# An attention and two MLP stages on one core: the odd heads' state product gets a bank of its own, the first unit full triangles, the range check two slots

## The reference, cut to what matters

```python
    for t in range(S):
        state = alpha[:, :, t, :, None] * state + np.einsum('bhd,bhe->bhde', k[:, :, t], v[:, :, t])
        y[:, :, t] = np.einsum('bhd,bhde->bhe', q[:, :, t], state)
...
    x = np.ascontiguousarray(attn_out.transpose(0, 2, 1, 3)).reshape(B, S, H * D)
...
    xn = (x - mu) / np.sqrt(var + 1e-06) * g_ln
    ch = np.maximum(xn @ w_ch1, 0.0) @ w_ch2
    return (x + ch).astype(np.float32)
...
    X = np.fft.fft(x, axis=1)
    X = np.fft.fft(X, axis=2)
    mixed = np.real(X).astype(np.float32)
    u = x + mixed
```

## Time and profile before

| what | value |
|---|---|
| median of 3 runs | 779.54 us (778.01 to 780.23) |
| profiled execution, its time | 780.88 us |
| its span in the trace | 779.4 us |
| PE busy | 765.5 us, 98% |
| DVE, ACT, POOL busy | 450.4, 218.6, 54.8 us |
| stage one (attention and first MLP) | up to about 440 us |

### The profile page before, as it was taken

One profiled execution on the slowest core, in us unless ns is written; L12 is line 12 of the kernel. 1 busy time (PEld: TensorE's weight loads), 2 busy tenths in 40 slices (PEclk: granted clock), 3 DMA queues, 4 the chain that ended last, 5 costly groups with the idle time before them and its releaser, 6 DMA issues.

```text
span 779.4 us, 17212 instructions
## 1 busy us (share of the span) xinstructions
PE 765.5 (98%) x7148; PEld 740.3 (95%) x7148; DVE 450.4 (58%) x1035; ACT 218.6 (28%) x453; POOL 54.8 (7%) x110
## 2 busy tenths in 40 slices
PE   7999999999999999999999999999999999999998
PEld 7889899999999999999999999999999999999998
DVE  6787777766666665675586865347434564342422
ACT  3453242232312323124243332212221223111221
POOL 1000000000000000000003100300012000300000
PEclk9899999999999999999999999999999999999999
DMA  9352304041130410443023511030003000000000
GB/s 248 99 151 66 97 33 139 32 108 61 52 88 32 119 62 32 138 144 113 21 92 102 193 51 55 27 102 31 1 32 102 30 0 30 0 0 31 1 31 30
DMA packets 29827, 54.10 MB, mean 69 GB/s; under 512 B 1916, under 2 KB 24700, under 8 KB 29756
## 3 DMA queue, kind: packets, MB, share of 16 engines
q1 hardware_dynamic: 29756, 53.10, 22.1%
HBM read 43.65 MB, written 13.37 MB: 73 GB/s over the span
## 4 chain that ended last, share of the span: by engine, by line
PE 89%; DVE 4%; issue 4%; ACT 1%; DMA 1%; POOL 0%; SPq 0%; POOLq 0%; DVEq 0%; ACTq 0%
PE h L97 13%; PE h L99 12%; PE acc L99 12%; PE h L98 12%; PE acc L97 12%; PE acc L98 12%; PE side_bank L1452 3%; PE side_bank L1463 2%; PE side_bank L1472 2%; PE side_bank L1402 2%; PE side_bank L98 2%; PE side_bank L99 2%; PE side_bank L97 1%; PE side_bank L1414 1%; PE side_bank L1385 1%
## 5 line engine op out<-in xcount | busy, mean ns | idle before, releaser
L171 DVE SCALAR_TENSOR_TENSOR hT_low<-h,hT_high 128x384 fp32r<-128x384 f32 (+1 forms) x204 | 108.5, 532 | 187.5 <-ACT hT_high L166 187.3
L97 PE MATMUL h<-xnT_high,w_high 128*128 128x384 f32 (+1 forms) x612 | 208.5, 341 | 1.2 <-DVE hT_low L171 0.9
L99 PE MATMUL h<-xnT_high,w_low 128*128 128x384 f32 (+1 forms) x612 | 199.9, 327 | 0.0
L98 PE MATMUL h<-xnT_low,w_high 128*128 128x384 f32 (+1 forms) x612 | 199.6, 326 | 0.0
L166 ACT ACTIVATE hT_high<-h 128x384 fp32r<-128x384 f32 (+1 forms) x204 | 96.4, 472 | 354.6 <-PE h L99 354.0
L97 PE MATMUL acc<-w_high,hT_high 128*128 128x384 f32 x576 | 194.3, 337 | 0.0
L99 PE MATMUL acc<-w_high,hT_low 128*128 128x384 f32 x576 | 193.3, 336 | 0.0
L98 PE MATMUL acc<-w_low,hT_high 128*128 128x384 f32 x576 | 192.8, 335 | 0.0
L97 PEld LDWEIGHTS h<-xnT_high,w_high 128*128 128x128 f32 x612 | 115.2, 188 | 5.7 <-issue 0.9
L98 PEld LDWEIGHTS h<-xnT_low,w_high 128*128 128x128 f32 x612 | 115.5, 189 | 0.0
L99 PEld LDWEIGHTS h<-xnT_high,w_low 128*128 128x128 f32 x612 | 115.2, 188 | 0.0
(11 more groups left out here) (135 smaller groups left out, 764.6 us busy)
## 6 DMA issues: line engine op xcount, KB each, us to landing
stage<-w_dram SPq DMA_DIRECT2D x24, 384.0 KB, 3.6
x_scratch<-x_unit SPq DMA_DIRECT2D x8, 576.0 KB, 3.0
a_in<-alpha_dram SPq DMA_DIRECT2D x6, 672.0 KB, 5.1
q_in<-q_dram SPq DMA_DIRECT2D x6, 672.0 KB, 7.4
k_in<-k_dram SPq DMA_DIRECT2D x6, 672.0 KB, 6.8
v_in<-v_dram SPq DMA_DIRECT2D x6, 576.0 KB, 3.8
xb<-x_scratch SPq DMA_DIRECT2D x4, 576.0 KB, 4.2
xb<-x_turned SPq DMA_DIRECT2D x4, 576.0 KB, 6.9
```

The source lines that it names most:

```text
L97: pe.matmul(out, wh, xh, start=start, stop=False)
L98: pe.matmul(out, wh, xl, start=False, stop=False)
L99: return pe.matmul(out, wl, xh, start=False, stop=stop)
L171: dve.scalar_tensor_tensor(out=self.hT[1][:, j % H_SLOTS, 0:u.cols], in0=self.hps[j % H_BANKS][:, 0:u.cols], scalar=0.0, in1=self.hT[0][:, ...
```

## The change

1. **Chunks of all units but the first.** The masked scores by v (now `outputs_within`) all go to bank BSC, and stand behind the increments, one slot earlier. The products of state and q (now `outputs_carried`) stay in the output slot, alone: even heads add to BSC, odd heads start in BY. ACT copies BSC in one instruction, and DVE adds BY to the odd heads (`add_odd`), which raises `x_odd`. Scores of the next chunk wait for it too. The first chunk of a sequence multiplies with the zero state, where it left that product out.
2. **First unit.** The chunk isn't halved: scores are 128 by 128 with a full triangle (`causal`), increments go to one bank, chunk 0 has no state product, and chunk 1 does its scores ahead of its transposes. `first_half_state` is gone.
3. **Range check** in two slots: `check_above` in `range_slot`, `check_below` in the slot after it, behind that slot's `copy_y`. The slot of ONE[1] becomes 5.
4. **DVE order.** For ONE[2] `mask` and `next_state` come ahead of `prepare`. In the last unit of stage one, `dve_low` of slot 0 comes ahead of the residual of the unit before.

```diff
-ONE[1].scores, ONE[1].increments, ONE[1].outputs, ONE[1].range_slot = (4, 7), (5, 8), (6, 9), 7
+ONE[1].scores, ONE[1].increments, ONE[1].outputs, ONE[1].range_slot = (4, 7), (5, 8), (6, 9), 5
...
-            probs = [sb1(f"probs{i}", [P, PAIRS, SUB]) for i in range(2)]
+            probs = [sb1(f"probs{i}", [P, PAIRS, P]) for i in range(2)]
...
+                if u.first():
+                    for two in range(2):
+                        op = act.activation(odd_even(to)[:, two, :, :], of_pairs(first_y_bank(two)[:, 0:PAIRS * D]),
+                                            ACT.Copy)
+                else:
+                    op = act.activation(to, bank[BSC][:, 0:DM], ACT.Copy)
...
                 if slot == u.range_slot:
-                    check_range(u)
+                    check_above(u)
+                if slot == u.range_slot + 1:
+                    check_below(u)
...
+            def add_odd(u, c):
+
+                dve.wait_ge(x_ready, u.base + c + 1)
+                odd = odd_even(x_rows(u)(c))[:, 1, :, :]
+                dve.tensor_tensor(odd, of_pairs(bank[BY][:, 0:PAIRS * D]), odd, ALU.add).then_inc(x_odd, 1)
...
-                if slot > 1:
+                if slot > 1 and u.n != 2:
                     prepare()
                 if slot in u.scores:
                     mask(u, u.scores.index(slot))
                 if slot in u.increments:
                     next_state(u, u.increments.index(slot))
-                if slot <= 1:
+                if slot <= 1 or u.n == 2:
                     prepare()
...
+                if slot in u.outputs:
+                    add_odd(u, u.outputs.index(slot))
                 if slot == u.rows_slot:
                     final_statistics(u)
...
+            m.dve_low(dve, ONE[-1], 0)
             m.dve_residual(dve, ONE[-2], x_rows(ONE[-2]))
...
+            def first_scores(c):
+                u = ONE[0]
+                pe.wait_ge(k_ready, c + 1)
+                pe.wait_ge(q_ready, c + 1)
+                if c > 0:
+                    pe.wait_ge(sc_masked, 2 * c)
+                for h in range(PAIRS):
+                    for two in range(2):
+                        op = pe.matmul(score_bank(u, two)[:, h * P:(h + 1) * P], k_div[HR[two], c, h, :],
+                                       q_mul[HR[two], c, h, :], start=True, stop=True)
+                op.then_inc(sc_summed, 1)
...
+            def outputs_within(u, c):
+                s = u.slot(c)
+                for head in range(H):
+                    cols = slice(head * D, (head + 1) * D)
+                    for sub in SUBS:
+                        op = pe.matmul(bank[BSC][sub, cols], probs[head % 2][sub, head // 2, 0:SUB], v_in[sub, s, cols],
+                                       start=head == 0, stop=False)
+                op.then_inc(y_begun, 1)
+
+            def outputs_carried(u, c):
+
                 s, g = u.slot(c), u.base + c
...
+                pe.wait_ge(u_read, g + 1)
+                pe.wait_ge(y_begun, g + 1 - ONE[0].size)
                 for h in range(PAIRS):
                     for i, sub in enumerate(SUBS):
...
-                            op = pe.matmul(y_bank(u, two)[sub, h * D:(h + 1) * D], q_mul[HR[two], s, h, sub],
+                            to = (bank[BSC][sub, 2 * h * D:(2 * h + 1) * D], bank[BY][sub, h * D:(h + 1) * D])[two]
+                            op = pe.matmul(to, q_mul[HR[two], s, h, sub],
                                            state[HR[two], (u.state_slot(c), MIDDLE)[i], h, :],
-                                           start=False, stop=h == PAIRS - 1)
+                                           start=two == 1 and h == 0, stop=h == PAIRS - 1)
...
                         increments(u, c)
+                        outputs_within(u, c)
                     if slot == u.outputs[c]:
-                        outputs(u, c)
+                        outputs_carried(u, c)
```

More of the change, by code:

```diff
@@ L474, in flat, with odd_even @@
             return tile.rearrange("p h t -> p (h t)")
+        def odd_even(rows):
+            return rows.rearrange("p (h two d) -> p two h d", two=2, d=D)
         def of_pairs(rows):
@@ L661, in token_by_token @@
                 wait_apart(x_ready, u.base + u.size)
+                wait_apart(x_odd, u.base + u.size)
                 wait_apart(s_ready, u.base + u.size + 1)
@@ L949, in _ @@
             dve.sem_inc(out_stored[1], 16)
+            dve.sem_inc(x_odd, ONE[0].size)
             dve.memset(zeros[:, :], 0.0).then_inc(zeros_done, 1)
@@ L1045, in next_state @@
                                   ALU.add).then_inc(half_ready, 1)
[L1046 removed]
+                dve.wait_ge(half_ready, g + 1 - ONE[0].size)
                 if u.last(c):
@@ L1050, in next_state @@
                     return
-                dve.tensor_tensor(state_sum[:, :, :], added(second_bank(u)), middle, ALU.add).then_inc(u_read, 1)
+                dve.tensor_tensor(state_sum[:, :, :], added(bank[BY]), middle, ALU.add).then_inc(u_read, 1)
                 dve.wait_ge(u_read, g + 1)
@@ L1320, in _ @@
             for j in range(JH):
-                m.dve_low(dve, ONE[-1], j)
+                if j > 0:
+                    m.dve_low(dve, ONE[-1], j)
                 for kind, k in SEQ_SLOTS_0.get(j, ()):
@@ L1429, in increments @@
                 wait_v(u, c)
-                if u.first():
-                    pe.wait_ge(u_read, g)
-                else:
-                    pe.wait_ge(sc_masked, 2 * g + 2)
+                pe.wait_ge(sc_masked, 2 * g + 2)
                 for h in range(PAIRS):
-                    for psum, rows in zip((bank[BKU], second_bank(u)), SUBS[:1] if u.last(c) else SUBS):
+                    for psum, rows in zip((bank[BKU], bank[BY]), SUBS[:1] if u.last(c) else SUBS):
                         for two in range(2):
@@ L1438, in increments @@
                 op.then_inc(u_summed, 1)
-            def outputs(u, c):
-                s, g = u.slot(c), u.base + c
-                wait_v(u, c)
-                pe.wait_ge(sc_masked, 2 * g + 2)
-                if u.first() and c > 0:
-                    pe.wait_ge(x_ready, g)
-                if not u.first():
-                    pe.wait_ge(u_read, g + 1)
-                for h in range(PAIRS):
-                    for two in range(2):
-                        cols = slice((2 * h + two) * D, (2 * h + two + 1) * D)
-                        for i, sub in enumerate(SUBS):
-                            op = pe.matmul(y_bank(u, two)[sub, h * D:(h + 1) * D], probs[two][sub, h, :],
-                                           v_in[sub, s, cols], start=h == 0,
-                                           stop=u.new(c) and i == 0 and h == PAIRS - 1)
-                op.then_inc(y_begun, 1)
-                pe.wait_ge(*((half_ready, g) if g else (first_half, 1)))
-                pe.wait_ge(y_begun, g + 1)
+            def outputs_within(u, c):
[6 more added lines that the diff above has]
+                op.then_inc(y_begun, 1)
@@ L1477, in attention_done @@
                 pe.wait_ge(x_ready, u.base + u.size)
+                pe.wait_ge(x_odd, u.base + u.size)
                 pe.wait_ge(u_read, u.base + u.size)
```

154 lines of the change are left out of this document (82 added, 72 removed).

## The result

The changed kernel takes **784.18 us** (median of 5 executions, 783.62 to 785.4); the kernel before took 778.08 beside it (777.42 to 780.23). The ratio, taken of the means, is **1.0073, interval 1.0055 to 1.0091**: slower, by 5.7 us (6.1 between the medians). The forecast was 770.4, with a range of 767.0 to 775.3 and 0.05 for slower. The profiled execution took 785.4, 1.2 above the median.

What follows compares the result with a forecast made beforehand. PE, busy 98% of the span, was taken as the bound. Terms -7.7 - 0.4 - 0.8 - 4.0 + 3.8 = -9.1 took the profiled 780.88 to 771.8, median 770.4 us; range 767.0 to 775.3.

Steps and rivals of the forecast that it cites:

- Range check in two slots: +3.8: Later loads of decays make DVE late and stall PE: 3.3 us for ONE[3], 0.5 for ONE[4] to ONE[7].
- The late issue itself: Unit of ONE[3]: the range check's second pass, which the decay load awaits, ends at 120.95 instead of 116.94 us.
- 0.5 for the four: Units of ONE[4] to ONE[7]: late decays cause no stall or a few tenths, 0.5 us for all four.
- Landing: Unit of ONE[3]: the decay load takes 5.1 us and lands at 126.1, so DVE stands 3.0 us.
- The clock: Unit of ONE[3]: PE's stall for late decays was counted as 2.3 us, with no lower clock behind it.
- (d): Rival: late decays stall every unit as they do ONE[3], +12.7 us instead of 0.5, total 783.1; chance 0.05.
- Blocks moved, -7.7: 22 chunks beside an MLP: moving masked scores by v behind the increments removes PE's 0.35 us pipeline wait each.
- rival (b): At the moved blocks the array's drain moves instead of going; 3.5 us won instead of 7.7, total 774.6; chance 0.12.
- `add_odd`, 0: DVE's extra addition per chunk and ACT's single copy cost nothing, bar 0.9 us charged for one late `x_odd`.
- DVE order, -0.4: Units 0 and 1: waits for `state_sum` and a mask go, less 0.9 and 0.2 us for late `x_odd`.
- First unit, -4.0: First unit: unhalved chunk, new order, no hole and full clock start the first MLP at 24.9 instead of 28.9 us.
- `dve_low`: Start of stage one's last unit: `hT_low` made before the residual ends PE's 0.66 us wait; -0.8 us.

Runs made afterwards that it cites:

- experiment 2: Kernel before with only the range check split into two slots (and its earlier slot beside unit 0): 792.65 us, ratio 1.0174.
- experiment 8: Changed kernel with SP issuing the load of the keys only once the decays have landed: 785.65 us, ratio 1.0076.
- experiment 13: Changed kernel with the split range check one slot earlier in the full units and beside ONE[2]: 771.18 us, ratio 0.9905.
- Experiment 7: Changed kernel, split kept, with the copy of turned rows behind the last values, the store of x rows and the first tables on SP: 775.46 us.
- experiment 6: Changed kernel with one slot for the range check, plus two additions of odd heads moved earlier on DVE: 771.1 us, ratio 0.9894.
- experiment 5: Changed kernel with one slot for the range check, plus the masked scores by v back in the output slot: 778.66 us, ratio 0.9995.
- experiment 10: Kernel before with only the new first unit: 777.17 us, ratio 0.9984.
- experiment 12: Kernel before, unchanged, profiled for another look at its first unit: 777.36 us.
- experiment 3: Changed kernel with the load of the last values ahead of the copy of turned rows on SP: 782.6 us, ratio 1.0036.
- experiment 4: Changed kernel with one slot for the range check and the last values loaded ahead of the turned rows: 777.34 us, ratio 0.9977.

## Why the prediction was wrong

The step that failed is the term **"Range check in two slots: +3.8"**. It costs 11.7 us in the changed kernel (784.18 against 772.45 with one slot) and 13.4 in the kernel before (experiment 2); against a split that begins one slot earlier it is 13.0 (784.18 against 771.18). The rest of the sum, forecast as -12.9, is some -7 (ratios 0.9909 and 0.9905). So the other terms together are off by some 6 us, of which below.

- *The late issue itself* was right. It was put at 20.7 us after the start of unit 2, and came at 20.6 (117.07). In the full units "0.5 for the four" was near: nothing in three of them, 0.95 in unit 6, and that only in this profile of three.
- *Landing.* I took the 5.1 us of the earlier trace rows as fixed. The decays took 6.6, and the stall was 3.84 instead of 2.3. The keys now leave within 0.9 us instead of 3.3 behind them; whether this made the difference stays open (experiment 8). A second look at the kernel before has 5.8 at the same place.
- *The clock.* I reckoned a stall at its own length, although show what followed the hole of 1.60 us. It cost 2.6 us in unit 2, and about as much in unit 7: the four blocks from L1435 took 0.64, 1.89, 3.05 and 2.11 us against 0.39, 1.04, 1.67 and 1.65, **2.9 us**.
- *What else is behind on the queue.* This is the largest part. The prediction followed one transfer, the decays, to its reader. Keys, turned rows, values and a store stand behind it on SP, and the last values had 0.4 us of slack. Unit 7 is 8.2 us longer than in experiment 13 (57.65 against 49.48). Experiment 7 wins the same 8.2 by the order on SP alone. I had written of (d), the rival on the slower side, that late decays "stall every unit"; the time it gave, 783.1, is near the result, but by another mechanism: three units stall, not all, and the dearest for values, not decays. That this number came near is luck.

The other terms:

- *Blocks moved, -7.7.* The mechanism and the 0.35 a chunk are right (0.37), and rival (b) is refuted. But the price holds in 15 of 22 chunks, 5.5 us; beside units 0 to 2 the other 7 chunks gave 1.1 instead of 2.45.
- *`add_odd`, 0, and DVE order, -0.4.* The late `x_odd` of ONE[2] was put at 0.9 and is 1.1, in unit 0 0.2 and is 0.4. Its cause is order: experiment 6 gets 1.35 back. Both terms together came to +1.6 in units 0 to 2 (experiment 5); in unit 2, 1.0 of it, PE has a new wait of 0.6 for `hT_low`. A busy share of 58% for DVE said nothing about these units.
- *First unit, -4.0.* The trace shows 3.5, from 28.88 to 25.36. But the second execution of the kernel before starts its first MLP at 25.73: 3.15 of the 3.5 are the longer hole and the half clock, which only a part of the executions of before have. The median won 1.2 (experiment 10). I made the sum against one profiled execution and took its 1.34 above the median as a constant; it was the very thing that the term claimed to remove. Piece by piece it went as worked out: scores 1.09 (1.05), masked scores by v 1.72 and 1.82 (1.6), state product 1.02 (0.8).
- *`dve_low`*, -0.8: 0.81.

What made the hole near 17.5 us is still open. It stood in the same block in the three profiles with the old first unit, 1.60 and 0.94 us long in the kernel before and 0.16 in experiment 2, between 1.3 and 2.9 us behind the first packet of the instruction queue, and doesn't appear in the new first unit. The Trainium skill (Runtime: NRT & Kernel Launch, Instruction fetch mechanics) gives PE a buffer of 2048 instructions; with it no fetch need be awaited so early. The runs don't decide it: no kernel shifted the instruction count alone. Open too is a store in stage two, `out_dram<-u_front` near 565 us, which took 3.0 us to land in the kernel before. It took 4.4 in the changed kernel, where it cost nothing, and 4.7 to 5.5 in all experiments that start from it, where one unit of stage two is 0.2 to 1.0 us longer.

## What to carry to other kernels

When a step moves later, follow everything that stands behind it on its queue up to each reader, and ask of each transfer how far ahead of its reader it lands: slack of 0.4 us looks the same in a list of waits as slack of 40. Price a stall of PE with the clock behind it, and compare a term against the executions' spread, not against one profile, above all a term for something that the profile names no cause for. Splitting work over two slots is fine if it begins a slot earlier.

## What the runs showed of the hardware

- After waits of PE of 0.9 and 1.1 us the granted clock stayed at 1.00 (experiment 12, unit 6 of the changed kernel; unit 7 of experiment 6), after 1.6, 2.1, 2.9, 3.8 and 5.2 us it fell to 0.50, which cost 2.6 us (after 3.8; 1.5 in experiment 7) and 2.9 us (after 5.2) on top of the wait. The length of the wait alone doesn't decide it: in the first unit it fell at 12.2 us in experiment 2 after waits of 0.57 and 0.76, and at 20.7 us in the profiled execution of experiment 10 without a wait.
- On one queue a 576 KB load took 3.7 us ahead of 1.1 MB of rows turned in small packets (experiment 3) and 23.0 us behind them (changed kernel), and a store behind them 14.4 (experiment 4) instead of the page's 3.0. From the landing of the keys ahead of these rows to that of the values behind them it took 23.1 to 24.6 us in seven profiles.
